# Attention on one core: the heads unrolled as one pipeline, values stationary, q and k transposed together

## The reference

```python
q_bits = (einsum('bhsd,dk->bhsk', q, proj) > 0)      # k_bits the same; bucket = sum of bits * 2**i
mask = q_bucket[:, :, :, None] == k_bucket[:, :, None, :]
scores = where(mask, matmul(q, k.T) / sqrt(64), -1e9)
attn = exp(scores - max(scores)); attn = attn / (sum(attn) + 1e-9)
x = matmul(attn, v)                                  # heads side by side: 1536 tokens x 512
g = where(h > 0, h, exp(min(h, 0)) - 1); y = g @ w_out    # h = x @ w_in, 512 -> 2048 -> 512
out = y + gate * (relu(y @ w1[e]) @ w2[e])           # best of 8 experts e, only where y @ w_skip > 0
```

## Time and profile before

| | us |
|---|---|
| median of 3 runs | 741.7 (740.39 to 743.52) |
| span of the profiled execution, first to last instruction | 738.4 |
| of it PE busy | 697.5 (94%) |
| DVE, ACT, POOL busy | 359.0, 286.2, 216.5 |

### The profile page before, as it was taken

The page is one execution under the profiler, slowest core; times in us unless marked ns, Lnnn a source line. Parts: engine busy times, 40 slices in busy tenths (PEclk is TensorE's granted clock), DMA queues, the critical chain, the costliest instruction groups (busy, mean ns, idle before and its releaser), DMA issues.

```text
span 738.4 us, 12482 instructions
## 1 busy us (share of the span) xinstructions
PE 697.5 (94%) x4416; PEld 646.5 (88%) x4416; DVE 359.0 (49%) x674; ACT 286.2 (39%) x509; POOL 216.5 (29%) x229
## 2 busy tenths in 40 slices
PE   5999999999999999999999999999998985999996
PEld 3899999899999999999999999998997964999986
DVE  8565666666676666622223222322224246545542
ACT  2444545454545454443333333333332321334330
POOL 3532555555555555244020002000003033111111
PEclk9898999999999999999999999999999996999999
DMA  4012222211112122100002000200066776699300
GB/s 115 16 46 62 61 61 60 60 50 49 52 59 60 60 60 61 26 2 15 0 1 87 1 1 0 85 0 0 0 243 215 254 234 207 221 332 331 124 10 24
DMA packets 44382, 61.76 MB, mean 84 GB/s; under 512 B 15812, under 2 KB 28100, under 8 KB 44352
## 3 DMA queue, kind: packets, MB, share of 16 engines
q1 hardware_dynamic: 43072, 57.70, 23.6%
q0 software_dynamic: 1280, 3.65, 1.5%
HBM read 53.50 MB, written 8.39 MB: 84 GB/s over the span
## 4 chain that ended last, share of the span: by engine, by line
PE 77%; DVE 15%; issue 6%; ACT 1%; DVEq 1%; POOL 0%; DMA 0%; POOLq 0%; ACTq 0%
PE banks L1258 18%; PE banks L1273 17%; PE banks L1202 10%; PE banks L1385 8%; DVE row_max_halves L817 7%; PE banks L1400 6%; PE banks L1190 6%; PE banks L1154 3%; PE banks L1147 3%; DVE row_max L826 1%; PE banks L1166 1%; PE banks L1291 1%; DVE g_lo L899 1%; DVE attn_sum L846 1%; PE banks L1183 1%
## 5 line engine op out<-in xcount | busy, mean ns | idle before, releaser
L1202 PEld LDWEIGHTS banks<-v_nat,probs 128*128 128x128 f32 x1152 | 167.8, 194 | 0.2 <-issue 0.2
L1202 PE MATMUL banks<-v_nat,probs 128*128 128x65 f32 x1152 | 161.1, 263 | 0.0
L1258 PE MATMUL banks<-x_hi,w_split 128*128 (+1 forms) x512 | 140.1, 335 | 0.0
L920 DVE SCALAR_TENSOR_TENSOR g<-exp_min_h,banks 128x384 f32<-128x384 f32 x64 | 35.5, 554 | 197.2 <-ACT exp_min_h L704 197.1
L1273 PE MATMUL banks<-w_split,g_hi 128*128 128x512 f32 x384 | 121.5, 397 | 4.8 <-DVE g_lo L899 4.8
L669 ACT ACTIVATE probs<-banks 128x768 f32<-128x768 f32 x96 | 77.9, 812 | 117.7 <-PE banks L1190 117.4
L817 DVE TENSOR_REDUCE row_max_halves<-banks 128x1 f32<-128x384 f32 x192 | 96.5, 545 | 10.2 <-PE banks L1166 10.0
L701 ACT ACTIVATE exp_min_h<-banks 128x384 f32<-128x384 f32 x64 | 31.5, 491 | 176.7 <-PE banks L1258 176.7
L1258 PEld LDWEIGHTS banks<-x_hi,w_split 128*128 128x128 f32 x512 | 93.5, 188 | 2.4
L1258 PE MATMUL banks<-x_lo,w_split 128*128 (+1 forms) x256 | 86.2, 337 | 0.0
L1273 PEld LDWEIGHTS banks<-w_split,g_hi 128*128 128x128 f32 x384 | 71.3, 190 | 16.9 <-DVE g_lo L899 6.0
(11 more groups left out here) (180 smaller groups left out, 996.5 us busy)
## 6 DMA issues: line engine op xcount, KB each, us to landing
expert_w<-in_moe_w SPq DMA_DIRECT2D x32, 1024.0 KB, 5.5
w_stage<-in_moe_w_in SPq DMA_DIRECT2D x16, 256.0 KB, 2.7
w_stage<-in_moe_w_out SPq DMA_DIRECT2D x16, 256.0 KB, 2.9
q_nat<-in_q SPq DMA_DIRECT2D x16, 192.0 KB, 2.9
k_nat<-in_k SPq DMA_DIRECT2D x16, 192.0 KB, 3.0
v_nat<-in_v SPq DMA_DIRECT2D x16, 192.0 KB, 3.0
out<-y SPq DMA_DIRECT2D x4, 768.0 KB, 4.0
y_rows<-y SPq DMA_DIRECT2D x4, 768.0 KB, 5.5
```

Source lines behind the costliest of these rows:

```text
L920: dve.scalar_tensor_tensor(gb[:, j % 2, :], e_neg[:, j % 2, :], -1.0, banks[:, j % 2, 0:BN], ALU.add, ALU.max).then_inc(s_["g_ready"], 1)
L1202: mm = pe.matmul(ps_o[:, t * V1:t * V1 + V1], probs[:, s % 3, t * P:t * P + P], v_nat[w][:, s, :], start=(s == 0 and t == 0), stop=(s == Q ...
L1258: mm = pe.matmul(banks[:, j % 2, 0:BN], w, x, start=(c == 0 and w is hi and x is x_hi), stop=(c == KC - 1 and w is lo))
```

## The change

It rewrites attention and what feeds it; the two later stages keep their code.

- All heads are written out, without a loop. `PSUM_ORDER` lists every use of PSUM in PE's order, and the uses take three slots of two banks in turn: a use waits until the use three places before it has been read (`take`, `consumed`). Scores now share these slots. Banks 6 and 7 hold the weighted sums.
- q and k of a head are loaded into one tile, [q | k] on 128 columns, two heads ahead, and transposed together: 6 transposes for 12. ACT rounds the result (`hi`), DVE makes the remainder (`lo`), each in one operation over 768 columns, and SP copies their halves into the rows of `qa`, `qb`, `ka`, `kb` by six DMAs within SBUF (`copy_rows`). Scaling by 1/8 moves into the exponential. These four tensors exist three times.
- The projection is one unit of 6 matmuls for q and k. Each half row of maxima becomes a whole one: 6 reductions of 768 instead of 12 of 384, and 96 rows are contracted instead of 128.
- Weighted sums: v (64 columns) beside 64 columns of ones is stationary, and `probs` moves, 384 columns, f32: 2 matmuls for each s instead of 6. The output arrives transposed, with the denominators in the other 64 rows. Odd heads have the two halves swapped, so a pair fills 128 rows.
- v is centred: its mean (now an f32 matmul of 384 columns and a DVE reduction) is taken off before and added after, which covers rows without a match.
- The denominators of a pair are loaded as [128, 12] (`load_den`), inverted by DVE, stored to DRAM and read back spread over 64 partitions each (`load_rden`); POOL multiplies and adds the mean (`normalise`). PE's output transposes and ACT's copies of them go.
- Weights are loaded in place, tiles 0 to 8 during heads 0 to 8 and tiles 9 to 15 after the last scores, beside the first feed-forward block, which waits for each tile. The splits of x for blocks 0 and 1 run on POOL in heads 10 and 11.

The core of the diff (the five loops over heads are those of SP, POOL, ACT, DVE and PE, in this order):

```diff
+def head_units(h, s):
+    a, b = h + 1, h + 2
+    plan = [[], [("MAX", a, 0), ("MAX", a, 1)], [("MAX", a, 2), ("MAX", a, 3)],
+            [("MAX", a, 4), ("MAX", a, 5), ("T", b, 0)], [("VSUM", b, 0), ("MAX_T", a, 0)], [("BITS", b, 0)]][s]
+    return [x for x in plan if x[1] < HEADS]
+FIRST_UNITS = [("T", 0, 0), ("BITS", 0, 0), ("T", 1, 0)] + [("MAX", 0, t) for t in range(QT)] + \
+              [("VSUM", 0, 0), ("MAX_T", 0, 0), ("BITS", 1, 0), ("VSUM", 1, 0)]
...
+            def load_qk(h):
+                if h >= 2:
+                    sp.wait_ge(s_["tq_done"], h - 1)
...
+            def copy_rows(h):
+                i = h % 3
...
+                sp.wait_ge(s_["hi_done"], h + 1)
+                for dst, src in ((qb[i][0:D, :], hi[0:D, :]), (kb[i][0:D, :], hi[D:P, :]),
+                                 (qa[i][D:P, :], hi[0:D, :]), (ka[i][0:D, :], hi[D:P, :])):
+                    sp.dma_start(dst.bitcast(F32), src.bitcast(F32)).then_inc(rows_copied[i], 16)
+                sp.wait_ge(s_["lo_done"], h + 1)
+                for dst, src in ((qa[i][0:D, :], lo[0:D, :]), (ka[i][D:P, :], lo[D:P, :])):
+                    sp.dma_start(dst.bitcast(F32), src.bitcast(F32)).then_inc(rows_copied[i], 16)
...
+            def load_rden(pair):
+                sp.wait_ge(s_["rden_stored"], 32 * (pair + 1))
+                if pair:
+                    sp.wait_ge(s_["xt_ready"], pair)
+                sp.dma_start(rden_rows[:, :], den_rows[2 * pair:2 * pair + 2, :].unsqueeze(1).broadcast_to([2, D, S]))\
+                    .then_inc(s_["rden_loaded"], 16)
...
+            for h in range(HEADS):
+                if h % 2 and h >= 3:
+                    store_rden(h // 2 - 1)
+                if h + 3 < HEADS:
+                    load_qk(h + 3)
+                if h + 1 < HEADS:
+                    load_mean(h + 1)
+                if 0 < h < EARLY:
+                    load_w(h)
+                if h % 2 and h >= 3:
+                    load_rden(h // 2 - 1)
+                if h % 2 == 0 and h:
+                    load_den(h // 2 - 1)
+                if h + 3 < HEADS:
+                    load_v(h + 3)
+                if h + 2 < HEADS:
+                    copy_rows(h + 2)
...
+            for h in range(HEADS):
+                if 0 < h < HEADS - 1:
+                    centre_v(h + 1)
+                if h < EARLY:
+                    split_w(h)
+                if h % 2 and h >= 3:
+                    normalise(h // 2 - 1)
+                if h in (10, 11):
+                    split_x(h - 10)
...
+            for h in range(HEADS):
                 for s in range(QT):
+                    if s == 4 and h + 2 < HEADS:
+                        round_qk(h + 2)
...
+                    act.activation(probs[:, n % 4, :].rearrange("p (b n) -> p b n", b=2), psum("SCORES", h, s), ACT.Exp,
+                                   scale=float(D) ** -0.5).then_inc(s_["exp_done"], 1)
+                    if s == 1 and h:
+                        outputs(h - 1)
...
+            for h in range(HEADS):
+                if h + 1 < HEADS:
+                    bits(h + 1)
+                    if h == 0:
+                        mean_of_v(1)
+                    for t in range(QT):
+                        maximum(h + 1, t)
+                    row_maxima(h + 1)
+                if h + 2 < HEADS:
+                    low_qk(h + 2)
+                    mean_of_v(h + 2)
+                if h + 1 < HEADS:
+                    minus_maxima(h + 1)
+                if h % 2 == 0 and h:
+                    inverse_den(h // 2 - 1)
...
+                elif kind == "MAX":
+                    if i == 0:
+                        pe.wait_ge(s_["bits_done"], h + 1)
+                        pe.wait_ge(rows_copied[h % 3], 96 * (h // 3 + 1))
...
+            def weighted(h, s, b):
+                n = QT * h + s
+                if b == 0:
+                    pe.wait_ge(s_["exp_done"], n + 1)
...
+                mm = pe.matmul(banks[:, 6 + b, 0:HALF], v_ones[h % 2][:, s, :], probs[:, n % 4, b * HALF:b * HALF + HALF],
+                               start=(s == 0), stop=(s == QT - 1))
...
+            for n in range(QT * HEADS):
+                h, s = n // QT, n % QT
+                scores(h, s)
+                units = head_units(h, s)
+                if n >= 2:
+                    weighted((n - 2) // QT, (n - 2) % QT, 0)
+                for unit in units[:1]:
+                    prepare(*unit)
+                if n >= 2:
+                    weighted((n - 2) // QT, (n - 2) % QT, 1)
+                for unit in units[1:]:
+                    prepare(*unit)
```

More of the change, by code:

```diff
@@ L52 @@
 BANK = 512
-V1 = D + 1
 INFO = 6
@@ L109, in build @@
         mxp = sb("row_max_pad", [P, P], F32)[0]
-        mx2 = sb("row_max_halves", [P, QT, 2], F32)[0]
         mx = sb("row_max", [P, QT], F32)[0]
[L112 to L116, removed]
+        average = sb("average", [P, P], F32)[0]
+        v_mean = [sb(f"v_mean{u}", [P, D], F32)[0] for u in range(2)]
@@ new lines, in load_mean, with load_den @@
+            def load_mean(h):
+                sp.wait_ge(s_["mean_ready"], h + 1)
+                u = h % 2
+                with nc.allow_non_contiguous_dma(reason="small"):
+                    sp.dma_start(mean_T[u * D:u * D + D, h // 2:h // 2 + 1], v_mean[u][0:1, :])\
+                        .then_inc(mean_loaded[h], 16)
+            def load_den(pair):
+                sp.wait_ge(s_["od_ready"], 2 * pair + 2)
+                if pair:
+                    sp.wait_ge(s_["rden_ready"], pair)
+                for u in range(2):
+                    row = D * (1 - u)
+                    sp.dma_start(den[:, u, :], o_den[(2 * pair + u) % 4][row:row + 1, :]).then_inc(s_["den_loaded"], 16)
@@ L322, in _ @@
+            load_qk(0)
             for half in range(2):
                 sp.dma_start(pj[half * D:half * D + D, :], proj).then_inc(s_["const_loaded"], 16)
+            load_qk(1)
+            load_v(0)
+            load_v(1)
+            copy_rows(0)
+            load_qk(2)
+            copy_rows(1)
+            load_mean(0)
+            load_w(0)
             with nc.allow_non_contiguous_dma(reason="small"):
@@ L370, in store_y @@
+            sp.wait_ge(s_["st_done"], QT * HEADS)
+            for j in range(EARLY, EARLY + 2):
+                load_w(j)
+            load_den(PAIRS - 1)
+            for j in range(EARLY + 2, EARLY + 4):
+                load_w(j)
+            store_rden(PAIRS - 1)
+            load_rden(PAIRS - 1)
+            sp.wait_ge(s_["xt_ready"], PAIRS)
+            for j in range(EARLY + 4, FT):
+                load_w(j)
             def store_y(n):
@@ L684, in g_high @@
+            outputs(HEADS - 1)
             def g_high(n, j):
@@ new lines, in _ @@
+            low_qk(0)
+            bits(0)
+            low_qk(1)
+            for t in range(QT):
+                maximum(0, t)
+            row_maxima(0)
+            mean_of_v(0)
+            minus_maxima(0)
+            for h in range(HEADS):
[3 more added lines that the diff above has]
+                        mean_of_v(1)
+                    for t in range(QT):
+                        maximum(h + 1, t)
[7 more added lines that the diff above has]
+                    inverse_den(h // 2 - 1)
@@ new lines, in scores @@
+            def scores(h, s):
+                i = h % 3
+                to = take("SCORES", h, s)
+                if s == 0:
+                    pe.wait_ge(s_["neg_done"], h + 1)
+                for b in range(2):
+                    half = slice(b * HALF, b * HALF + HALF)
+                    pe.matmul(to[:, b, :], ka[i][:, s * P:s * P + P], qa[i][:, half], start=True, stop=False)
+                    mm = pe.matmul(to[:, b, :], kb[i][:, s * P:s * P + P], qb[i][:, half], start=False, stop=True)
+                mm.then_inc(s_["st_done"], 1)
@@ L1249, in _ @@
+            for s in (QT - 2, QT - 1):
+                for b in range(2):
+                    weighted(HEADS - 1, s, b)
             pe.wait_ge(s_["gates_loaded"], 32)
```

751 lines of the change are left out of this document (285 added, 466 removed).

## The result

The changed kernel takes **718.35 us** (717.25 to 721.17, four runs) where the kernel before took 741.05 (739.66 to 743.52): 0.9704 of it, 95% interval 0.968 to 0.9728. The forecast was 710.3, with 718 to 737 for the third rival, in which part is given back. The profiled execution is 716.5 us long.

A forecast was written before the change was run, and what follows sets the result against it. PE's issued work was taken to bound attention: +1.1 - 2.3 + 14 x (16.95 - 19.09) - 0.2 = -31.4 us on the 738.4 span gives 707, plus 3.3 carried: 710.3 us. Forecast range 701 to 722; 8 in 10, 698 to 736.

The forecast's parts named there:

- the third rival: Attention: part given back by exposed loads (1.0 us a head) or the broadcast in six odd heads; 718 to 737; chance 0.13.
- the sign of the rivals: Trace sign against the forecast: PE idle before the maxima's first matmul with a DMA as its releaser.
- The head: Attention, per head: PE's issued work sums to 16.75 us, with 0.2 left for unlisted items, 16.95 against 19.09 before.
- the first rival: Weighted sums: f32 columns stream once, 0.173 us a record; PE about 12.6 a head, total near 655; chance 0.05.
- turning the operands saves nothing by itself: Weighted sums: 12 short records a step become 4 long ones that stream, 1.34 us for 1.26.
- Exposed loads: PE weight loads in attention: expected to go, covered by 0.335 us records; if they stay, 1.0 us a head is lost.
- The start: Before the first scores: maxima stand behind rounding, low parts and six copies; first scores at 21.9 us, +1.1.
- The copies' cover: Row copies in attention: landing at 17.2 to 18.0 us, first read at 20.15, leaving 2.2 us of cover.
- I take nothing for it: Broadcast of denominators (`load_rden`): issued some 2 us into an odd head, 1.2 to 17.8 us long, costed at zero.
- its two-engine case: Broadcast on two engines: 8.9 us, 1 us of cover; issued 2 us late, about 1 to 3 us per odd head.
- The second rival: Attention: row copies land late, 1.5 us wait then 3 us lost at half clock every head; 776 us; chance 0.10.
- the remaining 417 us are the same: Feed-forward layer and experts after attention: 417 us, expected unchanged.

The follow-up runs named there:

- run 5: Changed kernel with broadcast in two transfers and maxima waiting for their own two copies, plus weighted sums' operands turned back: ended at 798 us, a head 16.9 us.
- run 6: Changed kernel with broadcast in two transfers and maxima waiting for their own two copies, plus the six q and k transposes issued twice: 715.48 us.
- Run 1: Changed kernel with the broadcast of a pair's reciprocal rows issued as two transfers of outer dimension 64 instead of one of 2: 707.31 us.
- run 4: Changed kernel with weight tiles 3, 5 and 7 loaded and split one head later, the broadcast left as one transfer: 709.28 us.
- Run 10: On top of run 1, four more copies of 192 KB a head to tiles nobody reads, with the maxima waiting for all ten: 772.01 us.
- run 12: On top of run 11, the high part of the feed-forward input and small tiles behind it start 3136 bytes higher: 700.73 us.
- run 9: The changed kernel itself measured once more, with nothing altered: 719.85 us.
- runs 11: Changed kernel with spread broadcast, maxima's own copy wait and v summed on VectorE, plus separate tiles for the second head's split at the start: 701.72 us.

## Why the prediction was right, and what it missed

718.35 us lies in the forecast's range (701 to 722) and at the edge of the third rival's (718 to 737), and the trace has both: undisturbed heads as forecast, and PE idle before the maxima with a DMA as its releaser, which was the sign of the rivals. The heads are right by their mechanism. That the total came within 8 us is in part luck, since 6.4 us of gains that I had not forecast stand against 15.7 us of losses.

**The head.** Right, to 0.25 us: 16.75 summed, 16.95 forecast, 16.70 measured. A step of scores and sums takes 1.98 us (39.89 to 41.87 between first scores of steps), which is 4 x 0.173 and 4 x 0.322 for a record of 384 columns; I had 0.335, and the first rival's 0.173 is out. With 0.322 my sum is 16.4, so that 0.3 a head stands in none of its terms, 0.1 more than I had left for that. The Trainium skill (FP8 and Floating Point Precision, TensorE Precision Notes) says that true FP32 takes four passes, which makes two for each of the two records; 0.322 for 384 columns beside 0.173 for the fp32r one agrees. That turning the operands saves nothing by itself was right but for 0.2 (run 5). The rest of the 2.4 us came from fewer PE instructions and from what PE no longer waits for: no PE wait for a maximum is left in an undisturbed head, and run 6 shows that added PE work lengthens it one for one. Which part of the change removed which stall was not tried apart.

**Exposed loads.** I let them go; they are covered with the new orientation and there with the old one (run 5), so that step was right. The rival's price of 1.0 a head left out that the short records themselves take less: what shows in the end is 0.2.

**The start.** Forecast +1.1, measured +3.85. The term that was mis-sized is the copies: I had them landed at 12.2, they landed at 14.3. SyncE's issues follow each other every 0.64 us, not 0.5, and the last lands 3.9 us after its issue, not 2.7 to 3.0. The second head's low part waits for that, and the maxima behind it began at 16.10 and ended at 21.4 instead of 19.6. The rest is bits and means at half rate, 0.32 a record, for which I had allowed a part. The last copy's issue, the first maxima and VectorE's reductions of them:

```profile
10.36 0.60 SPq L315 DMA_DIRECT2D k_hi_lo_T<-qk_lo_T  x1
```

```profile
14.44 1.62 PE L1093 MATMUL banks<-k_hi_rows_T,q_hi_rows_T 96*128 96x384 f32 x4 [1.69 <-DMA k_hi_lo_T<-qk_lo_T]
```

```profile
16.10 5.27 DVE L770 TENSOR_REDUCE row_max<-banks 128x1 f32<-128x768 f32 x6
```

**The copies' cover.** I had 2.2 us; it is 0.7: in the head of first scores at 198.7 the last issue starts 15.4 us in, lands at 19.3, and the maxima begin at 20.0. The same two prices are the reason, and the maxima coming 0.2 earlier. In head 1 the cover was gone (a wait of 0.21). Six copies at 332 GB/s are also 3.6 us, not my 3.3; nothing hung on that.

```profile
214.06 0.60 SPq L315 DMA_DIRECT2D k_hi_lo_T<-qk_lo_T  x1
```

```profile
218.67 0.81 PE L1093 MATMUL banks<-k_hi_rows_T,q_hi_rows_T 96*128 96x384 f32 x2
```

**The broadcast.** "I take nothing for it" is the step that failed. The bounds were right, and so was the rival: its two-engine case with the issue late is what happened. The Trainium skill (DMA: Bandwidth & Descriptors, Why a DMA increments its semaphore by 16 and not by 1) gives two engines for an outer size of 2. Run 1 agrees: 11.9 us from issue to first use, against 3.8 to landing for the same bytes as two transfers of outer size 64. I set the issue at 2 us into the head, where the queue has it at 3.7, behind two stores, q, k, the mean and two weight loads, and I counted a cover of 0.7 us as 2.2. It hit three heads and not six, since I didn't see that weight loads end after head 8 (run 4). The rival priced them at 1 to 3 us each; they cost 1.9 to 4.0.

**The second rival** wanted 1.5 us of wait in every head and 3 us of clock. Run 10 gave it a case: 2.6 and 1.8, 772 us. The price for a wait was right as a sum and wrong in its parts. In the changed kernel's heads, waits of 1.63 to 1.89 us cost 0.3 on top of themselves, those of 2.21 to 2.37 cost 1.7. In run 10, waits of 1.98 to 3.39 us cost 1.5 to 1.9 on top in eleven of fourteen heads, 0.3 in one and 2.8 and 3.1 in two. The length of the wait alone doesn't decide it: in the kernel before, 1.56 us of idle time stood in a stretch at 0.55. So 2.6 us more of issues a head would have made the change a loss; a chance of 0.10 did not overrate that.

**Head 14** prepares the maxima of head 15, but there is no head 16 whose transposes, bits and mean it would make: 14.54, and I had counted it full. This windfall of 2.4 us hid a part of the miss.

**Behind attention**, "the remaining 417 us are the same" was wrong by 4.4: 0.8 is a wait of PE for VectorE at 300.52, where I had the last denominators "hidden" by 0.6 (their reciprocal held VectorE until 4.7 us into the block, not 3.6); 2.3 are the loop's 0.6 a block (run 12); 1.6 is the stretch of lower clock (run 9); the router and the experts took 0.2 less.

## What to carry to other kernels

A copy or load that many heads ahead look covered is covered only if its slowest part lands in time: before costing a transfer at nothing, look at how its outer dimension spreads and at what else shares its queue in that very stage, and let each reader wait for the pieces that it reads. Count PE's streamed columns, not its instructions, when an operand is turned; and when tiles move in SBUF, compare the period of a loop that was left alone.

## What was not expected of the hardware

The address of a tile changes a loop's rate: 70.94 us a block with the tile at its new place, 70.33 with it 3136 bytes higher, same instructions and no waits; the weight loads kept their 187 to 188 ns, and the matmuls' records grew by some 2 to 4 ns (337 for 335 in the products with x_hi, 396 for 393 in the down-projection's with g_lo). Which address rule is behind it stays open. A wait of about 2 us on PE is sometimes followed by a lower granted clock and sometimes not, at the same place of the program: in the last block of the feed-forward layer in 4 of 14 profiles (the two of the changed kernel and runs 11 and 12; waits of 1.91 to 2.20 us, against 1.76 to 2.07 in the others), and in one and in two of three heads in two profiles of the changed kernel. At the start, PE's fp32r matmuls came 0.32 us apart until 23.9 and 0.18 from 25.5 on, while the windows give the granted clock as 1.00 for all of that stretch.
